# Attention: the opening queue of SyncE handed out over ten head pairs

## What is computed

```python
scores = scale * np.matmul(q, k.transpose(0, 1, 3, 2))
thresh = np.max(scores, axis=-1, keepdims=True) - tau
scores = np.where(scores >= thresh, scores, -1000000000.0)
attn = exp(scores - max) / (sum + 1e-09)
attn_out = np.matmul(attn, v)
```

## Time and profile before

| what | value |
|---|---|
| three runs | 854.84, 855.4, 860.56 us; median 855.4 us |
| the profiled execution | 864.1 us |
| its span, first to last instruction | 862.0 us |
| mean granted clock of TensorE | 0.982 of full speed |
| attention | about the first 300 us of the span |
| DMA traffic | 123.78 MB, mean 144 GB/s |

### The profile page before, as it was taken

One profiled execution on the slowest core, in us unless ns is written; L12 is line 12 of the kernel. 1 busy time (PEld: TensorE's weight loads), 2 busy tenths in 40 slices (PEclk: granted clock), 3 DMA queues, 4 the chain that ended last, 5 costly groups with the idle time before them and its releaser, 6 DMA issues.

```text
span 862.0 us, 16594 instructions
## 1 busy us (share of the span) xinstructions
PE 824.7 (96%) x5209; PEld 693.0 (80%) x5210; DVE 444.4 (52%) x1041; ACT 382.3 (44%) x651; POOL 504.3 (59%) x461
## 2 busy tenths in 40 slices
PE   8869999999999987999999999999998999999998
PEld 5658878888887665788888888888787899998998
DVE  5748888888888875321221222122276445544522
ACT  3738878787887652121212221121375515424310
POOL 4646766676689736254989889997295505313100
PEclk9979999999999998899999999999999999999999
DMA  7977677768756167855555545562210111100101
GB/s 189 332 184 201 156 193 193 191 170 192 203 131 177 66 229 222 285 192 196 197 192 166 189 156 195 187 216 86 67 49 19 46 54 37 46 28 1 49 8 56
DMA packets 78982, 123.78 MB, mean 144 GB/s; under 512 B 26336, under 2 KB 39904, under 8 KB 78944
## 3 DMA queue, kind: packets, MB, share of 16 engines
q1 hardware_dynamic: 69200, 100.47, 40.1%
q0 software_dynamic: 3552, 11.54, 4.6%
q10 hardware_dynamic: 6192, 11.27, 3.9%
HBM read 70.63 MB, written 24.12 MB: 110 GB/s over the span
## 4 chain that ended last, share of the span: by engine, by line
PE 72%; POOL 8%; DVE 5%; DMA 4%; issue 4%; ACT 2%; another core or an unknown queue 1%; SPq 1%; ACTq 0%; DVEq 0%; POOLq 0%
PE psum L1404 14%; PE psum L1382 13%; PE psum L1798 12%; PE psum L558 7%; PE psum L616 6%; PE psum L1783 5%; PE psum L593 5%; PE psum L1813 3%; PE psum L1391 2%; POOL p_ring L353 2%; PE psum L626 1%; PE psum L1361 1%; POOL w_split L81 1%; PE psum L604 1%
## 5 line engine op out<-in xcount | busy, mean ns | idle before, releaser
L353 POOL TENSOR_SCALAR p_ring<-p_ring,xs_nat 128x576 f32<-128x576 f32 x144 | 105.6, 748 | 79.4 <-DVE xs_nat L461 79.4
L431 DVE TENSOR_REDUCE xs_nat<-psum 128x1 f32<-128x576 f32 x144 | 106.0, 750 | 47.3 <-PE psum L558 40.9
L558 PE MATMUL psum<-k_st,q_st 128*128 128x288 f32 x600 | 114.3, 317 | 11.4 <-issue 10.9
L446 DVE SCALAR_TENSOR_TENSOR p_ring<-psum,xs_nat,e_ring 128x576 f32<-128x576 f32 x144 | 114.6, 812 | 13.4 <-PE psum L604 8.9
L1382 PE MATMUL psum<-w_split,x_hi 128*128 (+1 forms) x352 | 118.1, 406 | 1.3 <-DVE x_lo L1503 1.3
L1286 POOL TENSOR_TENSOR w_split<-w_raw,w_split 128x1024 fp32r<-128x1024 f32 x48 | 114.9, 2394 | 4.0
L1404 PE MATMUL psum<-w_split,h_hi 128*128 (+1 forms) x352 | 116.6, 402 | 0.3 <-DVE h_lo L1508 0.3
L700 ACT ACTIVATE e_ring<-psum,xs_nat 128x576 f32<-128x576 f32 x144 | 105.5, 749 | 12.7 <-DVE xs_nat L431 12.0
L558 PEld LDWEIGHTS psum<-k_st,q_st 128*128 128x128 f32 x600 | 84.7, 190 | 22.7 <-issue 11.6
L718 ACT COPY p_t<-psum 128x512 f32<-128x512 f32 x144 | 84.3, 586 | 40.2 <-PE psum L593 37.2
L593 PE MATMUL psum<-ident,p_ring 128*128 128x128 f32 x576 | 87.8, 276 | 1.7 <-POOL p_ring L353 1.0
(11 more groups left out here) (200 smaller groups left out, 1588.9 us busy)
## 6 DMA issues: line engine op xcount, KB each, us to landing
w_raw<-w_dram SPq DMA_DIRECT2D x48, 512.0 KB, 3.5
k_st<-k_split SPq DMA_DIRECT2D x60, 320.0 KB, 5.4
q_st<-q_split SPq DMA_DIRECT2D x60, 144.0 KB, 2.5
xs_dram<-stage SPq DMA_DIRECT2D x23, 256.0 KB
ys_dram<-y_nat ACTq DMA_DIRECT2D x22, 256.0 KB, 2.1
xs_nat<-xs_dram ACTq DMA_DIRECT2D x21, 256.0 KB
k_nat<-k_t_dram SPq DMA_DIRECT2D x15, 320.0 KB, 4.3
out_dram<-out_sb SPq DMA_DIRECT2D x32, 144.0 KB, 1.8
```

Source lines behind the costliest of these rows:

```text
L353: pl.tensor_scalar(t, t, rsum[:, col:col + 1], 1.0, ALU.mult, ALU.mult).then_inc(s_norm, 1)
L431: dve.tensor_reduce(negmax[:, u % 3, 0:1], s_bank[u % 3][:, :, 0:HALF], AX.XY, ALU.max, negate=True).then_inc(s_max, 1)
L446: dve.scalar_tensor_tensor(out=p_tile[u].rearrange("p (a b) -> p a b", a=2), in0=s_bank[u % 3][:, :, 0:HALF], scalar=thresh[:, u % 3:u % 3 ...
L558: mm = pe.matmul(bank[:, x, 0:HALF], lhs, key[:, HALF * x:HALF * x + HALF], start=(j == 0), stop=(j == len(terms) - 1))
```

## The change

The four weight pieces and the thirteen transfers of `extra` leave the opening. They are issued behind the store of a pair instead:

| behind pair | what |
|---|---|
| 2, 3, 4, 5 | one weight piece each |
| 6 | both tables and the first store to `xs` |
| 7 | two stores to `xs` |
| 8, 9, 10, 11 | two stores to `ys` each |
| 12, 13 | one and three weight pieces, as before |

The loop over pairs 0 to 7 on SyncE becomes plain code. The programs of the other engines are the same.

```diff
--- before.py
+++ after.py
@@ -270,9 +270,6 @@
         load_v(1, 1)
         load_k(3, 1)
         load_q(3, 1)
-        for r in range(4):
-            load_w(r)
-        extra(sp)
 
         def pair(b, hp):
 
@@ -293,13 +290,12 @@
             sp.wait_ge(s_free, number(2 * b, hp, "r", 1) + 1)
             store_x(b, hp, m)
 
-        with sp.Fori(0, BATCH - 2) as b:
-            for hp in range(4):
-                pair(b, hp)
-        for p in range(4 * (BATCH - 2), PAIRS):
+
+        for p in range(PAIRS):
             pair(p // 4, p % 4)
-            for r in {PAIRS - 4: (4,), PAIRS - 3: (5, 6, 7)}.get(p, ()):
+            for r in {2: (0,), 3: (1,), 4: (2,), 5: (3,), PAIRS - 4: (4,), PAIRS - 3: (5, 6, 7)}.get(p, ()):
                 load_w(r)
+            extra(sp, p - 6)
 
     def pool(pl):
         def hold(semaphore, value):
@@ -2029,17 +2025,20 @@
                 s_zf, s_later, s_lg, s_free = sem("s_zf"), sem("s_later"), sem("s_lg"), sem("s_free")
                 LATER = 16 * (2 + XS_TILES - LEAST_TILES)
 
-                def for_later(sp):
-
-                    sp.dma_start(const[:], d["route_const"]).then_inc(s_later, 16)
-                    sp.dma_start(order, d["order_const"]).then_inc(s_later, 16)
-                    sp.wait_ge(s_zf, 1)
+                def for_later(sp, part):
+
+                    if part == 0:
+                        sp.dma_start(const[:], d["route_const"]).then_inc(s_later, 16)
+                        sp.dma_start(order, d["order_const"]).then_inc(s_later, 16)
+                        sp.wait_ge(s_zf, 1)
                     xs_spare = d["xs"][SLOTS * P:XS_TILES * P, :].rearrange("(a p) n -> a p n", p=P)
                     for j in range(XS_TILES - SLOTS):
-                        sp.dma_start(xs_spare[j], zeros[:, 0:DIM]).then_inc(s_later, 16)
+                        if part == (1 + j) // 2:
+                            sp.dma_start(xs_spare[j], zeros[:, 0:DIM]).then_inc(s_later, 16)
                     spare = d["ys"][LEAST_TILES * P:SLOTS * P, :].rearrange("(p r) n -> p (r n)", p=P)
                     for j in range(SLOTS - LEAST_TILES):
-                        sp.dma_start(spare[:, j * DIM:(j + 1) * DIM], zeros[:, 0:DIM]).then_inc(s_later, 16)
+                        if part == 2 + j // 2:
+                            sp.dma_start(spare[:, j * DIM:(j + 1) * DIM], zeros[:, 0:DIM]).then_inc(s_later, 16)
 
                 offset = [behind]
```

## The result

Over 20 executions of each kernel, the changed one has a median of 851.16 us (845.92 to 855.27) and the one before 855.59 us (851.58 to 860.75). The ratio is 0.9937, 95% interval 0.9917 to 0.9956: 5.4 us or 0.6% faster (the medians by themselves lie 4.4 us apart), where 10.9 us were forecast. A second comparison later gave 0.9908 (0.9874 to 0.9943), 7.9 us. The profiled execution took 849.1 us, with a span of 847.0 us.

What follows compares the result with a forecast made beforehand. PE bounds the kernel (busy 96% of the span), so only its waits for DMA or low clock can be won: 12.35 + 0.45 - 1.9 = 10.9 us off 855.4 gives 844.5 us, with 8 in 10 from 841.5 to 852.0.

Steps and rivals of the forecast that it cites:

- part 3: Transfers put behind pairs 2 to 11 cost what they delay, the next stack: 1.9 us, bounds 0 and 5.3.
- The hole: PE's wait before pair 2's scores: clearing the opening wins 12.35 us, 10.92 of it the hole; lower bound 9.9.
- SyncE's 8.3 us: In the opening: pair 2's stack began 8.3 us after it could have, SyncE issuing the block of transfers first.
- Pair 5 and the loop: Pair 5 was 0.48 us over the pace; plain code removes SyncE's address work there, counted as +0.45 us.
- Weight pieces behind 2 to 5: Cost of one piece ahead of each next stack: 0 to 0.3 us each, taken as 0.1, together 0.4.
- the row above: The weight piece behind pair 12: 1.9 us of slack used, 0.6 by issue and 1.3 by queue.
- 1.9 us of slack: Pair 13's stack, nothing in between: landed 11.5 us after pair 10's store, PE starting on it 13.4 us after.
- the 235.8 for pair 13's stack: Its landing time: last issue at 230.1 plus 5.7 us, 10.5 us after the first issue.
- the piece behind pair 12: Case in the trace before: stack landed 13.4 us after the store in place of 11.5, read as coming out even.
- SyncE's chain sets the pace: Rival: store, transfers, stack, scores form a ring; ten pairs lose 5 to 12 us, about 850 us; chance 0.15.
- a wait for `k_st` over 1 us: In pairs 5 to 14 of the profile after: the sign that SyncE's chain sets the pace.
- Zero stores and tables: Two stores behind each of pairs 7 to 11: 1.0 us, bounds 0 and 3.0; tables behind 6: 0.5, bounds 0 and 1.1.

Runs made afterwards that it cites:

- e3: The changed kernel with the four weight pieces back in the opening, tables and stores still spread; ratio to the kernel before 0.9914 (0.9882 to 0.9946).
- e8: e1 with the tables and zero stores put back in the opening; one run, attention 296.4 us, no ratio given.
- e7: The kernel before with SyncE's loop written out as plain code, nothing else changed; one run, attention 303.0 us, no ratio given.
- e2: The changed kernel with ys stores behind pairs 2 to 5 and weight pieces behind pairs 8 to 11; one run, attention 295.5 us.
- e4: The changed kernel with each weight piece of pairs 2 to 5 loaded as two 256 KB halves; one run, attention 295.8 us.
- e1: The changed kernel with the weight pieces of pairs 2 to 5 behind the pair's K load, not its store; ratio to before 0.9856.
- e5: The changed kernel with the weight pieces of pairs 2 to 5 behind the V loads, not the store; ratio to before 0.9868.
- e6: e1 with tables and zero stores also behind the K load; median 841.99 us, ratio to before 0.9825.
- e9: The changed kernel with each weight piece of pairs 2 to 5 issued just ahead of its pair's store; one run, attention 292.6 us.

## Why the prediction was wrong

The median of 851.16 us lies inside the stated 841.5 to 852.0, near its upper end, but the change is worth half to three quarters of what was forecast. What it wins came out as forecast; what it costs, part 3, was sized wrong.

**The hole, right.** 12.35 us were forecast for opening and low clock; the table has 12.6 gone, pair 2's stack issued at 27.09 and in time, pair 2 at 39.57. The cause as given, SyncE's time and the queue, was right too, and e3 and e8 put about half on each. The prediction had leaned on SyncE's 8.3 us; by e3 and e8 that is about half of the matter.

**Pair 5 and the loop, right in size, with some luck.** e7 shows 0.5 us there, for which 0.45 were counted. The cause given, the loop's address work, is a part of it, but by itself it makes nothing late: pairs 6 to 8 of the kernel before are in the loop too and in time. The rest is the packet on the `instruction` queue, which came too late to matter in e7.

**The step that failed: "Weight pieces behind 2 to 5: the row above is the nearest, same bytes; 0 to 0.3 us each, I take 0.1, together 0.4 us."** It was 5.3 us, over four times the upper bound of 1.2. The mechanism was named (a later stack against 1.9 us of slack), but both of its sizes were off. The slack is 1.4 us: the 235.8 for pair 13's stack was made with the median landing of two issues, and the last one landed at 236.0, after 5.9 us, so 11.8 us behind the store; PE starts 0.2 us after a landing. And a piece costs 2.5 to 3.0 us, 0.6 by the issue and 1.9 to 2.4 by the queue, in place of 1.9.

The price was carried over from one case, the piece behind pair 12, that differed in three ways: rows of 2 KB in place of 4 KB, no loads of Q and K behind the stack, and a place where PE was itself held up by POOL, so that an overrun would not have shown. The landing was 13.4 us after the store there, 14.5 here. That case was also not even. Its scores, those of pair 15, were due at 254.47 + 16.81 = 271.3, 13.1 us after their store, and the stack landed at 271.6. The scores began 1.2 us over the pace, with half of that named as a wait for POOL:

```profile
268.24 0.63 PE L593 MATMUL psum<-ident,p_ring 128*128 128x128 f32 x4 [0.61 <-POOL p_ring L353]
...
272.48 1.31 PE L558 MATMUL psum<-k_st,q_st 128*128 128x288 f32 x8
```

A case that comes out on the edge should have had a bound above it. And the rival "SyncE's chain sets the pace" had the right consequence, with 5 to 12 us for ten pairs; it was in fact four pairs at 1.3. The sign that the prediction had named for this rival, a wait for `k_st` over 1 us, is in the trace (1.07 at pair 5).

**Zero stores and tables.** 1.0 us was counted for the stores and 0.5 for the tables. The five pairs behind stores lost 0.02 us together: the first store drains while the second is issued, the lower bound. They are not free of risk, since they use up 1.1 us of slack: a stack that met a packet of the `instruction` queue behind them was 0.8 late in e2 and 0.5 in e4. The tables cost 0.3 and 0.2 in the changed kernel, but 1.5, 0.8, 0.4 and 0.5 in e1, e5, e3 and e4 with the same three transfers there. In e1 such a packet accounts for 1.2 of the 1.5; what varies in the others is open. e6 shows that it goes when they stand behind the K load.

**Why a piece costs more than two stores.** Shown: the kind decides (e2), being ahead of the stack decides (e1, e5), the order of store and piece decides in three of four pairs (e9), and loading in two halves with rows of half the length takes away a part (e4). The stack behind a pair of zero stores landed 12.8 us after the store, 1.1 us more than with nothing ahead, all of it SyncE's issuing. By the price of the Trainium skill's page "DMA: Bandwidth & Descriptors", section "Anatomy of one DMA — SWDGE (gpsimd) path", bytes over 436 GB/s for the moving part of one DMA, 512 KB are an estimated 1.2 us. The trace does not agree for either kind: the queue's part is 0 behind the stores and 1.9 to 2.4 us behind the pieces.

Argued only: that HBM reads queued right behind the 512-byte writes of the store are what is slow. The first forty packets took 339 to 629 ns behind the store (twelve pieces of three kernels) and 172 to 379 in the twenty pieces of e1, e5, e6, e8 and e9, which points there without proving it. Piece by piece it does not hold well. In e2 the pieces with 548 and 516 ns made their pairs 1.2 and 1.7 us late, those with 339 and 412 ns 0.9 and 0.6; but in the changed kernel 505, 602, 629 and 526 ns went with 1.3, 1.2, 1.1 and 1.6 us, and in its second profile 413 and 419 ns with 1.1 and 1.4. What makes a piece dear in the queue stays open beyond its kind, place, order and rows.

**The sum.** 12.6 + 0.5 won, 5.3 + 0.3 paid, gives 7.5 us; 10.9 were forecast, and 5.4 and 7.9 measured. Part 3 was counted at 1.9 us with bounds of 0 and 5.3; its 5.6 us in the trace are just beyond the upper bound, and nearly all of them are the term that was given 0.4.

## What to carry to other kernels

A transfer that nobody waits for still costs what it delays: put it behind the last urgent transfer of a period, not ahead of the first one of the next. Here the same bytes cost 5.6 us in one place and nothing in the other. When a slack is read off a trace, ask whether the case has the same direction, rows and followers, and whether the engine at that point would have shown an overrun at all. Slack is also what takes in disturbances that no line of the kernel shows, as the packets of the `instruction` queue here, so what is used up for a harmless transfer is missed later.

## What was new about the hardware

A 512 KB load from HBM right behind a store to HBM on the same queue had its first forty packets of 4 KB at 339 to 629 ns on average, and the others at 159 to 216; ahead of the store or behind other loads the first ones took 172 to 379. Two 256 KB stores of zeros in the same place delayed the transfers behind them by no more than their issue (10.7 us from first issue to last landing of the stack, with and without them). A stack on its way when a 16 KB packet of the `instruction` queue came, 1.6 to 4.0 us after its last issue, took 11.8 to 12.2 us in place of 10.5 to 10.9, in six of six cases without a piece ahead. SyncE took 4.90, 5.64, 7.18 and 6.53 us to issue the same eight stores (the two profiles of before, e7 and e8), so an issue has no fixed price; what sets it is open.
